# Laying a first MLP, cut into small pieces, under the attention of heads 9 to 32

## The chip, the cores and the metric

One core of a Trainium2 chip runs the whole program. The metric is device time in microseconds (us) of one execution. TensorE (PE) multiplies matrices and transposes, ScalarE (ACT) applies functions and copies, VectorE (DVE) does elementwise work and reductions, GpSimd (POOL) does slower elementwise work in SBUF, and SyncE (SP) issues the DMAs.

## The reference

Three stages follow one another. Heads are 32 (4 batches of 8), each 576 tokens by 64; the MLPs see 2304 tokens of 512.

```python
# attention, per head
scores = scale * (q @ k.T);  bias = -(cum[:, None] - cum[None, :])
scores = where(causal, -1e9, scores + minimum(bias, 0.0))
attn = exp(scores - max(scores));  attn = attn / (sum(attn) + 1e-9)
x = attn @ v                       # heads of a batch side by side: 512 wide
# first MLP (512 -> 1024 -> 512)
h = x @ w_in
solu = h * softmax(h)
ln = (solu - mean) / sqrt(var + 1e-6) * g_ln
x = ln @ w_out
# second MLP (512 -> 2048 -> 512)
h = x @ w_in2
g = h * clip(h + 3, 0, 6) / 6
out = g @ w_out2
```

Everything is float32 and is multiplied as split numbers: each operand is a high part (rounded to PE's fp32r type) and a low part (the rest), and a product is the sum of high*high, high*low and low*high, three matmuls.

## The kernel before, in words

The program has three stages, and each engine has its own instruction stream, written out by hand; semaphores with counts connect them.

**Attention** goes in steps of one head (`step(m, ...)` on every engine, loops over two heads). A head has five query tiles i of 128 rows (the last 64), and tile i has i+1 blocks of keys. In step m PE computes scores of head m+1 (`scores`, L483 high*high and low*high together through stacked q, L487 the causal mask, L489 the low part of k), transposes the probabilities of head m (`transpose_probs`, L502 and L504) and multiplies the transposed probabilities of head m-1 with the values (`weighted_values`, L523: for every key block three passes, v_hi with pT_hi, v_hi with pT_lo, v_lo with pT_hi; v is padded to 128 columns with zeros, so that two heads add up in one PSUM tile). DVE finds the row maximum while it adds the bias (L709), sums of exps get their epsilon (L731) and are inverted (L739), DVE scales the first four tiles of probabilities by them (`normalize`, L724), and makes the low part of the transposed probabilities (L718). ACT makes exps with their sums (L910), scales the last tile (L904), copies the transposed probabilities out of PSUM as the high part (L888), makes the high part of q and k (L894) and copies the finished pair of heads (L917). POOL makes the low parts of q and k (L399, L402), splits v (L408, L410), and w_in in 16 parts (L285, L287). SP loads q and k (L309), the bias row (L312) and v (L315, L316); every raw buffer is there twice, one for even and one for odd heads. Transposed probabilities go through PSUM banks 6 and 7 in turn, and scores through banks 0 to 3.

**First MLP**: 18 tiles of 128 tokens, in `slot(u, ...)`. For each tile ACT and POOL split x (L973, L427), PE makes h (`hidden`, 24 matmuls of 512 columns, L569 to L571) into one of two pairs of PSUM banks, DVE finds its maximum (L791), ACT the exps (L967), DVE the sum's inverse (L801, L804), the product (L806) and the mean (L810), ACT the squares (L961), POOL the inverse root (L433, L436), DVE the normalized rows (L796), PE transposes them (L580, 8 per tile), ACT and DVE split them (L978, L817), and PE projects three tiles at once (`project`, L594 to L596, 384 columns). ACT copies the result (L953).

**Second MLP**: 6 groups of 384 tokens, 16 pieces f each: 12 matmuls of 384 columns (L633 to L635) and 9 of 512 (L649 to L651) per piece.

What sets the order is the code itself: an engine takes its instructions in the order in which the functions issue them, and stands at the first one whose semaphore isn't there yet.

## Time and profile before

| | us |
|---|---|
| runs, median of 3 (lowest, highest) | 916.44 (915.82, 917.17) |
| profiled execution, its own span | 917.3 |
| PE busy | 866.4 (94%), 4864 matmuls |
| DVE busy | 446.7 (49%) |
| ACT busy | 429.9 (47%) |
| POOL busy | 243.6 (27%) |

The span lies within the spread of the runs, so nothing to speak of lies around it. PE's matmuls overlap: a row's duration reaches from an instruction's start to the modelled end of its result, and the next one starts earlier. How fast PE goes is seen from start to start. The busy shares are means over three stages: until 284 us attention, until 512 us the first MLP (with the first pieces of the second among its last tiles), then the second MLP.

### The profile page before, as it was taken

The page shows a single profiled execution, that of the slowest core. Times are in us where ns is not written, and L with a number is a line of the kernel's source. Part 1 is how long each engine was busy: PE and PEld are TensorE (multiplying, and loading weights), DVE is VectorE, ACT ScalarE, POOL GpSimd, SP SyncE. Part 2 cuts the span into 40 slices and gives each one's busy share as a digit, 9 for nine tenths or more (in the row PEclk, how much of TensorE's full clock was granted, in tenths as well). Part 3 has the DMA queues.
Part 4 walks back from the last instruction along what each step waited for, and adds up shares of the span by engine and source line. Part 5 has one row for each costly group of instructions (what it writes and reads, how often), then busy time and mean ns, then how long its engine had stood idle before and what let it go on. Part 6 is the DMA issues. An engine that isn't in the chain of part 4 may idle for free.

```text
span 917.3 us, 15385 instructions
## 1 busy us (share of the span) xinstructions
PE 866.4 (94%) x4864; PEld 766.0 (84%) x4864; DVE 446.7 (49%) x1146; ACT 429.9 (47%) x957; POOL 243.6 (27%) x259
## 2 busy tenths in 40 slices
PE   4988888998898999999999999999999999999997
PEld 3867777777777798998998999999898989999996
DVE  4888898888992835245244222232322332322222
ACT  4878888888883724334233343232322322322222
POOL 4456566665643314234210153000000000000000
PEclk9999999999999999999999999999999999999999
DMA  6955445454424000000000420000000000000000
GB/s 161 275 135 135 123 116 127 130 135 121 115 62 138 1 1 1 1 0 0 0 0 2 148 81 1 35 1 1 35 1 1 34 0 0 34 0 1 35 1 34
DMA packets 25744, 50.92 MB, mean 56 GB/s; under 512 B 5424, under 2 KB 9520, under 8 KB 25712
## 3 DMA queue, kind: packets, MB, share of 16 engines
q1 hardware_dynamic: 25712, 50.50, 19.8%
q8 instruction: 20, 0.33, 0.1%
q14 instruction: 12, 0.10, 0.0%
HBM read 45.69 MB, written 4.79 MB: 55 GB/s over the span
## 4 chain that ended last, share of the span: by engine, by line
PE 71%; ACT 10%; DVE 8%; issue 6%; DMA 2%; SPq 1%; ACTq 0%; DVEq 0%; POOL 0%; POOLq 0%
PE psum L650 7%; PE psum L651 7%; PE psum L635 7%; PE psum L633 7%; PE psum L634 7%; PE psum L649 7%; ACT prob L910 4%; PE psum L594 4%; PE psum L595 4%; PE psum L596 4%; PE psum L569 3%; PE psum L571 3%; PE psum L570 3%; ACT pT_hi L888 2%; DVE prob L709 2%
## 5 line engine op out<-in xcount | busy, mean ns | idle before, releaser
L845 DVE SCALAR_TENSOR_TENSOR act<-act,psum 128x384 f32<-128x384 f32 x96 | 53.1, 554 | 295.8 <-ACT act L1010 295.8
L1010 ACT ACTIVATE act<-psum,three 128x384 f32<-128x384 f32 x96 | 55.8, 582 | 269.0 <-PE psum L635 268.3
L910 ACT ACTIVATE prob<-prob,nmax 128x128 f32<-128x128 f32 (+4 forms) x160 | 96.0, 600 | 40.0 <-DVE nmax L709 40.0
L523 PE MATMUL psum<-pT_hi,v_sp 128*128 128x320 f32 (+3 forms) x448 | 101.3, 301 | 0.0
L709 DVE CUSTOM_DVE_ANT_0 prob<-psum,bias 128x128 f32<-128x128 f32 (+4 forms) x160 | 84.7, 531 | 9.3 <-DMA bias<-cum_dram 7.3
L483 PE MATMUL psum<-qk_st 128*128 128x128 f32 (+2 forms) x192 | 71.2, 379 | 10.6 <-POOL k_lo L402 10.6
L635 PE MATMUL psum<-x_hi,w_late_lo 128*128 128x384 f32 (+1 forms) x240 | 81.0, 337 | 0.0
L633 PE MATMUL psum<-x_hi,w_late_hi 128*128 128x384 f32 (+1 forms) x240 | 80.8, 337 | 0.0
L634 PE MATMUL psum<-x_lo,w_late_hi 128*128 128x384 f32 (+1 forms) x240 | 80.6, 336 | 0.0
L718 DVE TENSOR_TENSOR pT_lo<-psum,pT_hi 128x128 fp32r<-128x128 f32 (+4 forms) x160 | 77.2, 482 | 5.9 <-ACT pT_hi L888 3.2
L489 PE MATMUL psum<-k_lo,qk_st 128*128 128x128 f32 (+2 forms) x192 | 78.9, 411 | 0.0
L523 PEld LDWEIGHTS psum<-pT_hi,v_sp 128*128 128x128 f32 x448 | 76.3, 192 | 2.1
L502 PE MATMUL psum<-ident,prob 128*128 128x128 f32 x320 | 60.3, 288 | 17.5 <-DVE pT_lo L718 16.5
L399 POOL TENSOR_TENSOR qk_st<-qk_raw,qk_st 64x576 fp32r<-64x576 f32 x32 | 45.7, 1430 | 103.0 <-ACT qk_st L894 102.9
L888 ACT ACTIVATE pT_hi<-psum 128x128 fp32r<-128x128 f32 (+4 forms) x160 | 67.8, 424 | 9.4 <-PE psum L502 7.3
L651 PE MATMUL psum<-w_late_hi,g_lo 128*128 128x512 f32 x180 | 71.2, 396 | 0.0
L650 PE MATMUL psum<-w_late_lo,g_hi 128*128 128x512 f32 x180 | 71.1, 395 | 0.0
L649 PE MATMUL psum<-w_late_hi,g_hi 128*128 128x512 f32 x180 | 70.0, 389 | 0.0
L502 PEld LDWEIGHTS psum<-ident,prob 128*128 128x128 f32 x320 | 38.9, 146 | 35.5 <-issue 28.7
L523 PE MATMUL psum<-pT_lo,v_sp 128*128 128x320 f32 (+3 forms) x224 | 68.1, 304 | 0.0
L594 PE MATMUL psum<-lnT_hi,w_out_hi 128*128 128x384 f32 x192 | 64.7, 337 | 1.5 <-DVE lnT_lo L817 1.5
L724 DVE TENSOR_SCALAR prob<-prob,rden 128x128 f32<-128x128 f32 (+3 forms) x128 | 63.4, 496 | 2.3
(98 smaller groups left out, 2088.7 us busy)
## 6 DMA issues: line engine op xcount, KB each, us to landing
qk_raw<-qkT SPq DMA_DIRECT2D x64, 288.0 KB, 4.2
bias<-cum_dram SPq DMA_DIRECT2D x32, 288.0 KB, 4.1
out<-out_sb SPq DMA_DIRECT2D x6, 768.0 KB, 3.5
v_raw<-v_main SPq DMA_DIRECT2D x32, 128.0 KB, 2.0
w_late_raw<-w_in SPq DMA_DIRECT2D x10, 256.0 KB, 3.0
w_late_raw<-w_out SPq DMA_DIRECT2D x10, 256.0 KB, 3.8
w_in_raw<-w_in SPq DMA_DIRECT2D x1, 2048.0 KB, 12.3
w_out_raw<-w_out SPq DMA_DIRECT2D x1, 2048.0 KB, 15.4
```

The source lines that it names most:

```text
L502: last = pe.transpose(bank(ring)[:, j * P:(j + 1) * P], prob[s_ % 2][:, src * P:(src + 1) * P], ident[:, :])
L523: last = pe.matmul(psum[:, O_AT + q0:O_AT + q1], v_sp[p][:, j, v_part, :], pT[p][:, j, q0:q1], start=(p == 0 and k == 0), stop=(p == 1 and ...
L594: pe.matmul(ps, w_out_hi[:, f, cols], lnT_hi[:, f, :], start=(f == 0), stop=False)
L633: pe.matmul(ps, hi[:, cols], xh, start=(c_ == 0), stop=False)
L634: pe.matmul(ps, hi[:, cols], xl, start=False, stop=False)
L635: last = pe.matmul(ps, lo[:, cols], xh, start=False, stop=(c_ == NC - 1))
L649: pe.matmul(bank(4 + k), gh, hi, start=(f == 0), stop=False)
L650: pe.matmul(bank(4 + k), gh, lo, start=False, stop=False)
L651: last = pe.matmul(bank(4 + k), gl, hi, start=False, stop=(f == NF2 - 1))
L709: dve.tensor_tensor_reduce(out=prob[p][:, BLK[i] * P:BLK[i] * P + n], in0=psum[:, at:at + n], in1=bias[p][:, 0:n], scale=-SCALE, scalar=3. ...
L888: sc.activation(pT_hi[s_ % 2][:, 0:i + 1, i * P:i * P + width], ps, ACT.Copy).then_inc(pT_hi_done, 1)
L910: sc.activation(rows, rows, ACT.Exp, scale=-1.0, bias=nmax[:, p, i:i + 1], accum_out=rsum[:, p, i:i + 1]).then_inc(exp_done, 1)
```

## The change

- The attention's parts are now five slots to a head, n = 5m + k, and the first MLP is laid over the same numbering: tile t of it has the ten slots from 45 + 10t on (slot 45 is where the tenth head, m = 9, begins). Slots 0 to 159 hold attention, so tiles 0 to 11 begin beside it, and tiles 12 to 17 come behind it, in the same order of pieces. r = 0 to 9 is the slot within a tile. All loops are written out.
- h has one pair of PSUM banks instead of two, transposed probabilities one bank from slot 45 on, transposed rows and projections share one bank, and scores have three banks. The projection takes two tiles (256 columns) instead of three.
- The probabilities are not divided any more. v_hi and v_lo stand side by side as 128 columns, so a key block takes two passes (pT_hi, pT_lo) instead of three, and the output has the high product in one half of the partitions and the low in the other. ACT copies one half across (`copy_corr`), DVE adds the other (`add_parts`), POOL spreads the inverse sums over 64 columns (`widen`), PE transposes them (`scales`) and DVE multiplies a finished pair by them (`scale_pair`).
- q, k and v have one raw buffer each instead of two.

The diff is cut to the core: layout and numbering, the loads on SP, the spreading on POOL, then PE, DVE and ACT.

```diff
+SLOTS = 5
+TILE_SLOTS = 10
+MOE_FROM = SLOTS * (HEADS + 1)
+MOE_TO = MOE_FROM + TILE_SLOTS * NT
...
+CUTS = ((0, 2 * P), (2 * P, SEQ))
+SCORE_GROUPS = ((0, 1), (2,), (3,), (4,))
+SCORE_AT = (0, P, BANK, 2 * BANK, 2 * BANK - 288 - 512)
+PJW = 2 * P
+NPJ = NC * (NT // 2)
+H_CUTS = (0, 5, 10, 15, 20, 24)
...
-        qk_raw = [sb(a, f"qk_raw{p}", [P, 2, SEQ]) for p in range(2)]
-        v_raw = [sb(a, f"v_raw{p}", [P, NQ, DH]) for p in range(2)]
+        qk_raw = sb(a_region, "qk_raw", [P, 2, SEQ])
+        v_raw = sb(a_region, "v_raw", [P, NQ, DH])
...
+        O_BANK = 4
+        H_BANK = 5
+        L_BANK = 7
+        h_ps = psum[:, H_BANK * BANK:H_BANK * BANK + F1]
+        def turn(m, i):
+            n = SLOTS * m + i
+            return 3 if n % 2 == 0 or n >= MOE_FROM else L_BANK
...
+            def load_qk(h):
+                wait(sp, q_lo_done, h)
+                wait(sp, k_lo_done, h)
...
+            for m in range(-1, NH):
+                if 2 <= m + 2 < NH:
+                    load_bias(m + 2)
+                if m + 3 < NH:
+                    load_qk(m + 3)
+                if m + 2 < NH:
+                    load_v(m + 2)
...
+            def widen(h):
+                pool.wait_ge(rden_done, h + 1)
+                wait(pool, scale_ready, 2 * (h // 2))
+                pool.tensor_copy(wide[:, :, h % 2, :], rden[:, h % 2, :].unsqueeze(2).broadcast_to([P, NQ, DH])).then_inc(wide_done, 1)
...
+            def transpose_probs(m, i):
+                pe.wait_ge(exp_done, NQ * m + i + 1)
+                n = SLOTS * m + i
+                wait(pe, pT_lo_done, n if n >= MOE_FROM else n - 1)
...
+                q0, q1 = CUTS[c]
+                keys = [j for j in range(NQ) if j * P < q1]
+                for j in keys:
+                    at = max(q0, j * P)
+                    for part, (pA, pB) in enumerate(((pA_hi, pB_hi), (pA_lo, pB_lo))):
+                        pT = pB[:, j, at - q0:q1 - q0] if c else (pA[:, 0:2 * P], pA[:, 2 * P:3 * P])[j]
+                        last = pe.matmul(psum[:, O_BANK * BANK + at - q0:O_BANK * BANK + q1 - q0],
+                                         v_sp[h % 2][:, j, :, :].rearrange("p a d -> p (a d)"), pT,
+                                         start=(j == 0 and part == 0), stop=(j == keys[-1] and part == 1))
+                last.then_inc(pv_done, 1)
...
+            for n in range(-SLOTS, MOE_TO):
+                m, k = n // SLOTS, n % SLOTS
+                t, r = (n - MOE_FROM) // TILE_SLOTS, (n - MOE_FROM) % TILE_SLOTS
+                if 0 <= m < NH:
+                    transpose_probs(m, k)
+                if k < 4 and m + 1 < NH:
+                    scores(m + 1, k)
+                if k == 1 and 1 <= m <= NH:
+                    weighted_values(m - 1, 1)
+                if k == 3 and 0 <= m < NH:
+                    weighted_values(m, 0)
+                if t >= 0:
+                    if r in (1, 2) and t >= 1:
+                        transpose_ln(t - 1, r - 1)
+                    if r < 5:
+                        hidden(t, r)
+                    if 3 <= r < 9 and t >= 2:
+                        project(2 * (t - 2) + (r - 3) // 3, (r - 3) % 3, 3)
+                if k in (0, 2) and m % 2 == 0 and 2 <= m <= NH:
+                    scales(m // 2 - 1, k // 2)
...
+            def add_parts(h, c):
+                row, col, tok = tokens(h)
+                q0, q1 = CUTS[c]
+                dve.wait_ge(corr_done, 2 * h + c + 1)
+                x = xT[row:row + DH, col, tok + q0:tok + q1]
+                dve.tensor_tensor(x, psum[row:row + DH, O_BANK * BANK:O_BANK * BANK + q1 - q0], x, ALU.add).then_inc(sum_done, 1)
...
+            for n in range(-SLOTS, MOE_TO):
+                m, k = n // SLOTS, n % SLOTS
+                t, r = (n - MOE_FROM) // TILE_SLOTS, (n - MOE_FROM) % TILE_SLOTS
+                if m + 1 < NH and k >= 1:
+                    for i in SCORE_GROUPS[k - 1]:
+                        row_max(m + 1, i)
+                if 0 <= m < NH:
+                    split_probs(m, k)
+                    if k == 0:
+                        invert(m)
+                if k == 1 and 1 <= m <= NH:
+                    add_parts(m - 1, 1)
+                if k == 3 and 0 <= m < NH:
+                    add_parts(m, 0)
+                if t >= 0:
+                    if r in (1, 2) and t >= 1:
+                        split_ln(t - 1, r - 1)
+                    if r == 5:
+                        max1(t)
+                    if r == 6:
+                        solu(t)
+                    if r == 8:
+                        norm(t)
+                    if t == 0 and r < NF1:
+                        split_w_out(r)
+                    if t == NT - 1 and r in (3, 4, 7, 9):
+                        split_x2(0, (3, 4, 7, 9).index(r))
+                if k in (0, 2) and m % 2 == 0 and 2 <= m <= NH:
+                    scale_pair(m // 2 - 1, k // 2)
...
+            for n in range(-2 * SLOTS, MOE_TO):
+                m, k = n // SLOTS, n % SLOTS
+                t, r = (n - MOE_FROM) // TILE_SLOTS, (n - MOE_FROM) % TILE_SLOTS
+                if 0 <= m < NH:
+                    copy_probs(m, k)
+                if k == 0 and m + 2 < NH:
+                    split_qk(m + 2)
+                if 0 <= m + 1 < NH and k >= 1:
+                    for i in SCORE_GROUPS[k - 1]:
+                        exp_row(m + 1, i)
+                if k == 1 and 1 <= m <= NH:
+                    copy_corr(m - 1, 1)
+                if k == 3 and 0 <= m < NH:
+                    copy_corr(m, 0)
+                if t >= 0:
+                    if r in (1, 2) and t >= 1:
+                        copy_ln(t - 1, r - 1)
+                    if r == 5:
+                        exp1(t)
+                    if r == 7:
+                        square(t)
+                    if t >= 2 and r in (6, 9):
+                        copy_x2(2 * (t - 2) + r // 9)
+                    if t == 0 and r < NF1:
+                        split_w_out(r)
+                    if t == NT - 1 and r in (3, 4, 7, 9):
+                        split_x2(0, (3, 4, 7, 9).index(r))
+                if t >= -1 and r == 9 and t + 1 < NT:
+                    split_x(t + 1)
```

Three places of the instruction order, with their semaphore waits.

**DVE, attention with the heads one after another, before.** L709 is the row maximum, L724 the scaling of probabilities, L718 the low part of the transposed ones.

```order
L709 ISA prob,nmax<-psum,bias 128x256 [waits scores_ready]
L709 ISA nmax 128x1
L735 REGISTER_ALU
L61 REGISTER_ALU [waits den_done]
L739 RECIPROCAL rden<-den 128x2 [waits norm_last_done,norm_done]
L724 TENSOR_SCALAR prob<-prob,rden 128x512 [waits rden_done]
L714 REGISTER_ALU
L718 TENSOR_TENSOR pT_lo<-psum,pT_hi 128x2x128 [waits pT_hi_done]
```

and **after, from slot r = 6 of a tile on.** L667 is `add_parts`, L691 to L699 are `solu`, L640 is the row maximum, L651 the low part, L675 `scale_pair`.

```order
L667 TENSOR_TENSOR xT<-psum,xT 64x320 [waits corr_done]
L691 TENSOR_SCALAR den<-esum 128x1 [waits exp1_done]
L693 RECIPROCAL rden<-den 128x1 [waits den1_done]
L695 SCALAR_TENSOR_TENSOR es,solu_sum<-psum,rden,es 128x1024 [waits rden1_done]
L699 TENSOR_SCALAR neg_mu<-solu_sum 128x1 [waits solu_done]
L640 ISA prob,nmax<-psum,bias 128x384 [waits scores_ready]
L640 ISA nmax 128x1
L651 TENSOR_TENSOR pB_lo<-psum,pB_hi 128x3x128 [waits pT_hi_done]
L675 TENSOR_TENSOR xT<-psum,xT 128x320 [waits sum_done,scale_ready]
L640 ISA prob,nmax<-psum,bias 128x512 [waits scores_ready]
```

The scalings (L724) are gone; between the row maxima and low parts of the attention now stand the addition, which waits for ACT's copy, and the first MLP's `solu`, which waits for ACT's exps.

**PE, transposes and scores, before.** L502 and L504 are transposes of probabilities, L523 the product with the values.

```order
L483 MATMUL psum<-qk_st 128x128 [waits max_done]
L487 MATMUL psum<-mask_bf,ident_bf 128x128
L489 MATMUL psum<-k_lo,qk_st 128x128
L61 REGISTER_ALU [waits norm_last_done]
L504 MATMUL psum<-ident,prob 128x64 [waits pT_lo_done]
L504 MATMUL psum<-ident,prob 128x64 x4
L523 MATMUL psum<-pT_hi,v_sp 128x64
L523 MATMUL psum<-pT_lo,v_sp 128x64
L523 MATMUL psum<-pT_hi,v_sp 128x64
```

and **after, over the end of slot r = 9 of a tile and r = 0 of the next.** L465 are transposes of probabilities, L451 to L455 scores, L512 is `hidden`.

```order
L465 MATMUL psum<-ident,prob 128x64 [waits pT_lo_done,exp_done]
L465 MATMUL psum<-ident,prob 128x64 x4
L465 MATMUL psum<-ident,prob 128x128 [waits pT_lo_done,exp_done]
L451 MATMUL psum<-qk_st 128x128 [waits max_done,k_lo_done,q_lo_done]
L453 MATMUL psum<-mask_bf,ident_bf 128x128
L455 MATMUL psum<-k_lo,qk_st 128x128
L451 MATMUL psum<-qk_st 128x256
L453 MATMUL psum<-mask_bf,ident_bf 128x128
L455 MATMUL psum<-k_lo,qk_st 128x256
L512 MATMUL psum<-w_in_hi,xs_hi 128x512 [waits sq_done,xs_lo_done]
```

Nothing stands between two transpose groups there, and each waits (pT_lo_done) for the low part of the group just before it; behind the scores comes the next tile's first `hidden`, which waits for POOL's part of x (xs_lo_done).

**SP, the loads of a head, before:**

```order
L309 ISA [waits qk_lo_done]
L309 DMA qk_raw<-qkT 64x1152 x2
L61 REGISTER_ALU
L312 ISA [waits max_done]
L312 DMA bias<-cum_dram 128x576
```

and **after:**

```order
L286 DMA bias<-cum_dram 128x576 [waits max_done]
L282 DMA qk_raw<-qkT 64x1152 [waits k_lo_done,q_lo_done]
L282 DMA qk_raw<-qkT 64x1152
L290 DMA v_raw<-v_main 128x256 [waits v_lo_done]
L291 DMA v_raw<-v_tail 64x64
```

They look alike, but with one buffer the load of head h now waits for POOL's split of head h-1, where it waited for that of head h-2.

## Rows read from the trace of the kernel before

**Rows 1.** Windows in attention and second MLP: us, busy (instructions) per engine, clock, DMA share, GB/s

```profile
core 0: us, PE busy (x) PEld busy (x) DVE busy (x) ACT busy (x) POOL busy (x), PEclk, DMA share, GB/s
150.00:200.00 50.00, 44.91 (x328) 37.39 (x327) 44.61 (x140) 42.04 (x108) 30.66 (x32) 1.00 0.48 124
...
700.00:800.00 100.00, 100.00 (x504) 90.57 (x503) 29.28 (x56) 28.51 (x58) 0.00 (x0) 1.00 0.04 16
```

**Rows 2.** Timeline of one head: start us, us, engine, line, operation [idle before]

```profile
151.24 0.57 ACT L888 ACTIVATE pT_hi<-psum 128x512 fp32r<-128x512 f32 x1
...
152.74 1.16 ACT L894 ACTIVATE qk_st<-qk_raw 128x1152 fp32r<-128x1152 f32 x1
152.80 0.74 DVE L709 CUSTOM_DVE_ANT_0 prob<-psum,bias 128x576 f32<-128x576 f32 x1
...
153.47 0.48 DVE L718 TENSOR_TENSOR pT_lo<-psum,pT_hi 128x320 fp32r<-128x320 f32 x1
...
153.89 0.28 PE L523 MATMUL psum<-pT_lo,v_sp 128*128 128x192 f32 x1
...
153.97 1.53 POOL L399 TENSOR_TENSOR qk_st<-qk_raw,qk_st 64x576 fp32r<-64x576 f32 x1 [2.34 <-ACT qk_st L894]
154.00 0.33 PE L523 MATMUL psum<-pT_hi,v_sp 128*128 128x192 f32 x2
...
154.78 0.74 DVE L731 TENSOR_SCALAR den<-rsum 128x2 f32<-128x2 f32 x1 [0.35 <-ACT prob L910]
...
155.57 1.54 POOL L402 TENSOR_TENSOR k_lo<-qk_raw,qk_st 128x576 fp32r<-128x576 f32 x1
```

**Rows 3.** Groups by form, exps: busy us, mean ns | idle before

```profile
L910 ACT ACTIVATE prob<-prob,nmax 128x512 f32<-128x512 f32 x32 | 22.7, 710 | 0.0
...
L910 ACT ACTIVATE prob<-prob,nmax 128x128 f32<-128x128 f32 x32 | 12.7, 397 | 4.2 <-DVE nmax L709 4.2
```

**Rows 4.** Timeline, second MLP: PE from start to start

```profile
700.38 0.39 PE L649 MATMUL psum<-w_late_hi,g_hi 128*128 128x512 f32 x1
...
700.61 0.40 PE L650 MATMUL psum<-w_late_lo,g_hi 128*128 128x512 f32 x1
```

**Rows 5.** Tile qk_raw, 120 to 200 us: issue to landing

```profile
DMA to landing us min/median/max: 3.5/4.2/4.6
```

**Rows 6.** Timeline: first bias load; SP's answer to POOL

```profile
10.07 0.82 SPq L312 DMA_DIRECT2D bias<-cum_dram  x2
...
157.79 0.87 POOL L410 TENSOR_TENSOR v_sp<-v_raw,v_sp 128x320 fp32r<-128x320 f32 x1
...
158.91 0.34 SPq L315 DMA_DIRECT2D v_raw<-v_main  x1
```

**Rows 7.** Page, DMA issues: KB, us to landing

```profile
w_in_raw<-w_in SPq DMA_DIRECT2D x1, 2048.0 KB, 12.3
```

**Rows 8.** Timeline, the first MLP's chain in two tiles

```profile
341.02 0.14 DVE L801 TENSOR_SCALAR den<-esum 128x1 f32<-128x1 f32 x1
...
341.50 1.28 DVE L806 SCALAR_TENSOR_TENSOR solu<-psum,rden,e_sb 128x1024 f32<-128x1024 f32 x1
...
346.33 0.62 ACT L973 ACTIVATE xs_hi<-xT 128x512 fp32r x1
...
347.22 1.30 POOL L427 TENSOR_TENSOR xs_lo<-xT,xs_hi 128x512 fp32r<-128x512 f32 x1 [6.96 <-ACT xs_hi L973]
...
351.34 1.23 DVE L791 TENSOR_REDUCE nmax<-psum 128x1 f32<-128x1024 f32 x1 [2.58 <-PE psum L571]
...
352.60 1.12 ACT L967 ACTIVATE e_sb<-psum,nmax 128x1024 f32<-128x1024 f32 x1 [3.54 <-DVE nmax L791]
```

**Rows 9.** Timeline: PE around two gaps

```profile
311.41 0.39 PE L571 MATMUL psum<-w_in_hi,xs_lo 128*128 128x512 f32 x1
...
313.68 1.60 PE L580 MATMUL psum<-ident,solu 128*128 128x128 f32 x8 [1.89 <-DVE lnT_lo L817]
...
496.36 0.44 PE L594 MATMUL psum<-lnT_hi,w_out_hi 128*128 128x384 f32 x1 [1.48 <-DVE lnT_lo L817]
```

**Rows 10.** Window behind the first of these gaps

```profile
312.00:318.00 6.00, 4.32 (x16) 3.61 (x17) 5.34 (x10) 4.47 (x9) 2.55 (x4) 0.72 0.01 1
```

More of the change, by code:

```diff
@@ L37 @@
 KW = [min((i + 1) * P, SEQ) for i in range(NQ)]
+ROWS = [min(P, SEQ - i * P) for i in range(NQ)]
 INV_SCALE = float(DH) ** 0.5
@@ new lines, in build, with weight_chunk @@
+        xs_lo = sb(first, "xs_lo", [P, NC, P], F32R)
+        first.close()
+        a_region.close()
+        second = ExitStack()
+        w2_hi = [None] * NF2
+        w2_raw = [None] * NF2
+        w2_lo = [None] * NF2
+        def weight_chunk(f):
+            w2_hi[f] = sb(second, f"w2_hi{f}", [P, WT], F32R)
+            with nc.sbuf_tensor(f"w2_raw{f}", [P, WT], F32) as raw:
+                w2_raw[f] = raw
+            w2_lo[f] = sb(second, f"w2_lo{f}", [P, WT], F32R)
+        for f in range(EARLY):
+            weight_chunk(f)
@@ new lines, in scales @@
+            def scales(pair, c):
+                pe.wait_ge(wide_done, 2 * pair + 2)
+                pe.wait_ge(sum_done, 4 * pair + 3 + c)
+                q0 = CUTS[c][0]
+                tiles = ((0, 1), (2, 3, 4))[c]
+                for i in tiles:
+                    w = ROWS[i]
+                    at = O_BANK * BANK + i * P - q0
+                    last = pe.transpose(psum[:, at:at + w], wide[0:w, i, :, :].rearrange("p a d -> p (a d)"), ident[0:w, 0:w])
+                last.then_inc(scale_ready, 1)
@@ new lines, in hidden @@
+            def hidden(t, part):
+                if part == 0:
+                    if t == 0:
+                        pe.wait_ge(w_in_split, W_IN_PARTS)
+                    pe.wait_ge(xs_lo_done, t + 1)
+                    wait(pe, sq_done, t)
+                for n in range(H_CUTS[part], H_CUTS[part + 1]):
+                    half, c_, term = n // 12, n % 12 // 3, n % 3
+                    x = (xs_hi, xs_hi, xs_lo)[term][:, c_, :]
+                    w = (w_in_hi, w_in_lo, w_in_hi)[term][:, c_, half * BANK:(half + 1) * BANK]
+                    last = pe.matmul(bank(H_BANK + half), x, w, start=(n % 12 == 0), stop=(n % 12 == 11))
+                if part == len(H_CUTS) - 2:
+                    last.then_inc(h_ready, 1)
@@ new lines, in transpose_ln @@
+            def transpose_ln(t, part):
+                if part == 0:
+                    pe.wait_ge(ln_done, t + 1)
+                    pe.wait_ge(pT_lo_done, MOE_FROM)
+                    wait(pe, x2_done, min(2 * max(t - 1, 0), NPJ))
+                wait(pe, lnT_lo_done, 2 * t + part)
+                for j in range(4):
+                    f = 4 * part + j
+                    last = pe.transpose(bank(L_BANK)[:, j * P:(j + 1) * P], es[t % 2][:, f * P:(f + 1) * P], ident[:, :])
+                last.then_inc(lnT_ready, 1)
@@ new lines, in project @@
+            def project(q, part, parts):
+                g, d = q // NC, q % NC
+                if part == 0:
+                    if q == 0:
+                        pe.wait_ge(w_out_lo_done, NF1)
+                    pe.wait_ge(lnT_lo_done, 4 * (g + 1))
+                    if q % 2 == 0 and q < NPJ - 4:
+                        pe.wait_ge(lnT_lo_done, 2 * (q // 2 + 2))
+                    wait(pe, x2_done, q)
+                cols = slice(d * P, (d + 1) * P)
+                for n in range(24 * part // parts, 24 * (part + 1) // parts):
+                    f, term = n // 3, n % 3
+                    w = (w_out_hi, w_out_hi, w_out_lo)[term][:, f, cols]
+                    x = (lnT_hi, lnT_lo, lnT_hi)[term][g % 2][:, f, :]
+                    last = pe.matmul(bank(L_BANK, PJW), w, x, start=(n == 0), stop=(n == 23))
+                if part == parts - 1:
+                    last.then_inc(x2_ready, 1)
@@ L859, in copy_out @@
                 dve.tensor_copy(out_sb[:, 1, :], bank(5)).then_inc(out_copied_dve, 1)
-            def group(g):
+            for g in range(NG):
                 for f in range(NF2):
```

971 lines of the change are left out of this document (368 added, 603 removed).

## The prediction

> **What bounds the kernel now.** I read the windows first, then timelines. In attention [rows 1] PE, DVE and ACT are all busy 84 to 90% of the time and none is full, so the order in which they hand work on sets the pace; in the second MLP PE alone is full. The 504 matmuls of that window are 24 pieces of 21, so a piece takes 100/24 = 4.17 us. A head has 53 matmuls (12 for scores, 5 masks, 15 transposes, 21 products), so the 328 of the first window are 6.2 heads, 8.1 us each. The timeline of one head [rows 2] shows how to cost the two middle engines. DVE's row maximum lasts 0.74 but the next instruction starts 0.67 behind it: each DVE or ACT instruction takes about 0.1 less than its duration from its own engine, while another engine waits for all of it plus 0.03 to 0.12. An exp takes its full mean, 0.40 to 0.71 for 128 to 512 columns [rows 3], since a read of its sum follows.
>
> **What PE gains.** Two passes instead of three remove 7 of 21 matmuls a head. A matmul of 192 columns or less takes 0.11 us from start to start [rows 2]; in proportion up to the 0.23 of 512 columns [rows 4], 256 takes 0.12 and 320 takes 0.145. The products fall from 2.65 to 1.77 us a head, 28 us over 32 heads. A head needs 6.0 us of PE then (transposes 1.57, scores with masks 2.39, products 1.77, scales 0.27). A tile of the first MLP needs 24 x 0.23 (hidden), 8 x 0.105 (transposes) and 48 x 0.12 (projection in 256 columns, before 32 of 384 at 0.175), 12.0 us. Two heads and a tile would take 24.0 us if PE were never idle; before, they take 2 x 8.1 + 12.0 = 28.2 (24 x 0.23, 32 x 0.175 and 8 x 0.105 make 12.0, PE full). So there are 4.2 us to win for each tile that is overlaid, 48 for eleven and a half, if nothing new waits.
>
> **First heads, alone: slower.** With one raw buffer, loading and splitting q and k is a ring: ACT's copy 1.16, hand-over 0.07, POOL 1.43 and 1.54 with 0.17 between [rows 2], landing 4.2 after its issue, 3.5 to 4.6 [rows 5], SP's answer 0.25 behind POOL and 0.56 for the first of two issues [rows 6]: 9.4 us a head. The chain of DVE and ACT alone gives 8.1, so the ring decides. The first bias issue is at 10.07 [rows 6]; q and k of head 1 follow at 10.5 to 11.1, land at 15.3, and one ring later, 24.7, the first regular head begins. Nine heads take 84.6. The two weights of 2 MB, 12.3 us each to landing [rows 7], fall into this stretch on the same queue; between nothing and 12 each I take 5 together, since POOL's splitting of w_in waits too. Slot 45 comes at 24.7 + 84.6 + 5 = 114.3. At 8.1 a head it would come 12 sooner.
>
> **Tile and two heads overlaid.** I follow one tile's ten slots from the start of the first transposes. *First part, 2.66 us:* ACT is still at the exp of slot 9 (0.28 more), copies a projection (0.28) and splits x (0.62), POOL takes 0.07 + 1.29 and PE 0.12 more [rows 8]; `hidden` waits for that, and all behind it. *Second, PE's own work to slot 5, 13.15:* hidden 5.5, transposes of probabilities 1.46, scores 1.7, products 1.76, transposed rows 0.84, projection 1.9. *Third, slots 5 to 9, 13.76:* here ACT and DVE wait for each other. Transposes and copy 0.6, low part 0.21, inverses 0.42, maximum of h 1.26, exp of h 1.10, copy 0.29, two exps 0.89, the copied half 0.45, addition 0.40, `solu` 1.9 (0.14, 0.16, 1.28 and hand-overs), row maximum 0.59, exp 0.62, squares 1.14, copy 0.47, exp 0.71, half 0.39, addition 0.33, norm 0.72, row maximum 0.67, low part 0.60 [rows 2, 3, 8]; an operation without a row of its own is scaled by its columns from the rows of its engine, an estimate. The sum passes ACT's copy of the half into DVE's addition, behind which the next row maximum stands, and from there back to ACT's exp: four times in five slots. PE has 9.3 us of work there and waits for the rest, with gaps of about 1.4, 2.0 and (in the first part) 1.85 us. A tile is 29.6.
>
> **Two surcharges.** The small scaling of sums on DVE lasted 0.74, ending as POOL's instruction ended [rows 2], where the first MLP's equal lasts 0.14 with POOL idle [rows 8]. In slot 6 the same kind of instruction meets POOL's splits: 0.6 more, 30.2. The Trainium skill (SBUF — State Buffer, Who interferes with whom) says that GpSimd and VectorE share a port pair as an exclusive lock; with that rule the row agrees. PE's clock was full in 150 to 200 us [rows 1], with short gaps. After a gap of 1.9 us (start to start 2.27) eight transposes took 1.60, which is the 1.2 GHz level; after 1.48 the next matmul took 0.44, the 2.4 GHz level [rows 9]. The 6 us around the first had a mean of 0.72, which costs 6 x 0.28 = 1.7 us [rows 10]. Gaps here lie at that border, so I take half, 0.75 a tile, between 0 and 1.7. The Trainium skill (TensorE: Matmul & The Clock Gate, A second HAM failure mode) warns of a PE that idles briefly between groups and pays at each return to full clock; by it every tile would pay, 15 x 1.7 = 26 instead of 11.
>
> **The first two tiles** have no projection, but DVE and ACT split w_out (8 parts of 0.6): 51 for both. Tiles 2 to 10 take 9 x 30.95 = 278.6. Tile 11's first half runs beside the last head, 15.8, the rest 8.5.
>
> **Tiles 12 to 17, alone.** One pair of banks for h makes a ring. Hidden, transposed rows, the first projection piece, a wait of 0.4 for the shared bank and the matmul's own latency make 8.0 (5.5 + 0.84 + 0.95 + 0.4 + 0.3); then come maximum 1.26, exp 1.10, copy of a projection 0.38 (it stands behind the exp) and 0.1, three projection pieces 2.85 and 0.2, copy 0.28, split of x 0.62 and 1.48 on POOL: 16.3, where PE has 12.0 and before, with two pairs of banks, takes no more than that. PE's gap before the next hidden is 2.6. Six of them 97.8, clock 4.5, less 2.6 at the last.
>
> **Second MLP.** 96 x 4.17 = 400.3, then four projections (96 x 0.12), the last tile's transposes and their wait, 13.7 (before, this stood in the first MLP), and 5.5 for the last outputs, as now. Three edits I cost at nothing. The widening on POOL is hidden by POOL's idle time, 39% of the window [rows 1]; without it, it would lengthen the ring by its own 0.6 us. The transposed scales are counted in PE's 6.0. The splits of the late weights each stand beside a piece of 4.17 us, as before; if they came late, PE would wait for the seventh piece.
>
> **Sum.** 114.3 + 51 + 278.6 + 15.8 + 8.5 + 99.7 + 400.3 + 13.7 + 5.5 = 987 us, against the span of 917.3; the median of the runs lies 0.9 below it, so 986.
>
> **Rivals.** (1) *Faster:* ACT and DVE run ahead far enough in the single streams that PE stays full. The mechanism is the filling of slots 5 to 9 (PE idle 4.5 there) and of the wait for x. For it: DVE is busy 0.89 of 8.1 us a head [rows 1], 14.5 for two, and the tile adds some 5.5 [rows 8], so of 30 us it has 10 free. Against it: each wait named above is in instruction order. Both stretches at PE's 24.0 and 12.5 give 986 - 9 x 6.95 - 6 x 4.5 = 897. It decides from 25.5 us for an overlaid tile and 13.5 for a lone one; from there the kernel is faster than before. The Trainium skill (Perfetto Trace Analysis, Optimization Strategy) says that regimes with different contended engines may gain by interleaving; that is this rival. (2) *Half of the waits gone* (27 and 14.5 a tile, ring of 8.8): 986 - 36 - 11 - 5 = 934. (3) *Clock low in most of each tile's first part:* PE's 13.15 and 8.0 grow by a third or more, 986 + 9 x 3.5 + 6 x 3 = 1035. For it: the gap row; against it: attention at full clock with gaps. (4) That it doesn't do what it says: the order shows the pieces interleaved and two passes, so no chance.
>
> **How the numbers follow.** Forecast 55%, half of the waits 15%, clock 18%, faster 12%. The forecast's own bounds: 3.5 to 4.6 for landing (7 us), weights 0 to 24, clock 0 to 1.7 a tile, 1 us either way in an overlaid tile (10) and in a lone one: 955 to 1020. The range of 8 in 10 reaches to half of the waits and to the middle of the clock case: 922 to 1030. A measurement of this kernel can tell 0.2%, 1.8 us, from no change; hardly any case lies within it: faster 0.11, same 0.02, slower 0.87.
>
> **What would show it.** Right: attention rings of 9.4 us and slot 45 near 114 us; ACT waiting for DMA before its copy of q and k; an overlaid tile near 30 us with PE waiting for DVE's low parts and for POOL's part of x; a lone tile near 16 with PE waiting for `sq_done` and POOL; mean clock below 1.00 there. Wrong: PE full from slot 45 on, or the first heads at 8 us.

## The result, and the profile after

| | before | after |
|---|---|---|
| median of the runs, us | 916.52 | 1034.18 |
| profiled execution, span | 917.3 | 1036.5 |
| PE / DVE / ACT / POOL busy | 866 / 447 / 430 / 244 | 904 / 425 / 436 / 247 |

The changed kernel is slower: ratio 1.1265, 95% interval 1.121 to 1.132, about 116 us. The forecast was 986 with 922 to 1030; the direction was right, the time 48 us too low and just outside the range. The four runs spread from 1027.1 to 1038.6 us, and the profiled one is the slowest of them, so its stretches are at the long end.

Windows of the changed kernel: first heads alone, as [rows 1], tiles overlaid, lone tiles, second MLP.

```profile
core 0: us, PE busy (x) PEld busy (x) DVE busy (x) ACT busy (x) POOL busy (x), PEclk, DMA share, GB/s
27.00:117.00 90.00, 70.22 (x405) 59.03 (x403) 51.57 (x164) 59.04 (x151) 56.45 (x77) 0.79 0.54 146
150.00:200.00 50.00, 39.77 (x201) 32.31 (x202) 28.13 (x73) 28.35 (x69) 18.41 (x22) 0.73 0.24 63
200.00:450.00 250.00, 216.75 (x1365) 188.43 (x1362) 141.23 (x376) 141.29 (x343) 82.50 (x98) 0.89 0.24 63
...
508.00:600.00 92.00, 70.40 (x419) 60.01 (x418) 27.12 (x47) 25.12 (x49) 35.27 (x42) 0.96 0.07 25
700.00:800.00 100.00, 100.00 (x504) 90.67 (x503) 28.29 (x56) 28.25 (x58) 0.00 (x0) 1.00 0.05 16
```

No engine is full before the second MLP. In 150 to 200 us PE went through 6.6 matmuls a us before, at a granted clock of 1.00, and goes through 4.0 now, at 0.73; many of those of now are longer, so the busy share, 90% before and 80% now, is the fairer comparison. The second MLP is what it was, 504 matmuls in 100 us.

ACT's copy of q and k begins each head, so its starts are a ruler: head 2, slot 45, the ends of tiles 0 and 1, and the start of tile 10; then the exps of h of the first two lone tiles.

```profile
24.62 1.16 ACT L787 ACTIVATE qk_st<-qk_raw 128x1152 fp32r<-128x1152 f32 x1 [4.90 <-DMA qk_raw<-qkT]
...
119.66 1.15 ACT L787 ACTIVATE qk_st<-qk_raw 128x1152 fp32r<-128x1152 f32 x1
...
158.28 1.15 ACT L787 ACTIVATE qk_st<-qk_raw 128x1152 fp32r<-128x1152 f32 x1
...
189.04 1.15 ACT L787 ACTIVATE qk_st<-qk_raw 128x1152 fp32r<-128x1152 f32 x1
...
452.70 1.15 ACT L787 ACTIVATE qk_st<-qk_raw 128x1152 fp32r<-128x1152 f32 x1
...
523.34 1.11 ACT L831 ACTIVATE es<-psum,nmax 128x1024 f32<-128x1024 f32 x1 [4.86 <-DVE nmax L686]
...
540.04 1.11 ACT L831 ACTIVATE es<-psum,nmax 128x1024 f32<-128x1024 f32 x1 [4.83 <-DVE nmax L686]
```

Set against the prediction's sum (the second MLP's first matmul starts at 615.0):

| stretch | predicted | measured | difference |
|---|---|---|---|
| to head 2 | 24.7 | 24.6 | -0.1 |
| nine heads alone, with weights | 89.6 | 95.0 | +5.4 |
| tiles 0 and 1 | 51 | 69.4 (38.6 + 30.8) | +18.4 |
| tiles 2 to 9, eight | 8 x 30.95 | 8 x 32.96 | +16.1 |
| tile 10 to the second MLP | 155.0 | 162.3 | +7.3 |
| second MLP | 419.5 | 421.5 | +2.0 |

Together +49.1 on 987. How an overlaid tile goes is seen in tile 6. First PE at its start, the timeline:

```profile
319.31 0.30 PE L465 MATMUL psum<-ident,prob 128*128 128x128 f32 x1 [1.68 <-DVE pB_lo L651]
...
321.85 0.80 PE L512 MATMUL psum<-w_in_hi,xs_hi 128*128 128x512 f32 x1 [1.52 <-POOL xs_lo L399]
322.44 0.63 PE L512 MATMUL psum<-w_in_lo,xs_hi 128*128 128x512 f32 x1
322.87 0.63 PE L512 MATMUL psum<-w_in_hi,xs_lo 128*128 128x512 f32 x1
...
328.73 0.39 PE L512 MATMUL psum<-w_in_lo,xs_hi 128*128 128x512 f32 x1
328.96 0.39 PE L512 MATMUL psum<-w_in_hi,xs_lo 128*128 128x512 f32 x1
...
338.12 0.27 PE L465 MATMUL psum<-ident,prob 128*128 128x128 f32 x1
```

Then the chain of waits from the first transposes of slot 5 (start us, us, what):

```profile
338.27 0.12 PE psum L465
...
339.24 1.20 DVE nmax L686
...
340.46 0.55 ACT es L831
...
342.83 0.44 ACT xT L814
...
343.29 0.50 DVE xT L667
...
344.20 1.30 DVE es L695 x2
```

Both gaps of PE were forecast: one behind DVE's low part, one behind POOL's part of x. After them a matmul of 512 columns goes from start to start in 0.43 us (322.44 to 322.87) until about 327.8, then in 0.23 (328.73 to 328.96), as in [rows 4]: 5.9 us at the 1.2 GHz level, which at half speed is 3.0 us lost. From `hidden` to slot 5 PE takes 16.3 us (321.85 to 338.12), where 13.15 were forecast. The chain from slot 5 on passes maximum, exp, ACT's copied half, DVE's addition and `solu` in the forecast order.

### The profile page after: what moved, and what is told of

Same layout as the page of the kernel before. It is cut to its first block, busy times and chain, and to the rows that moved or that the text cites. A ratio compares the mean times of both kernels' runs of the same rounds, so it can differ in the third digit from the quotient of the medians.

```text
span 1036.5 us, 13705 instructions
## 1 busy us (share of the span) xinstructions
PE 904.2 (87%) x5008; PEld 793.6 (77%) x5008; DVE 425.2 (41%) x1038; ACT 436.2 (42%) x985; POOL 247.4 (24%) x291
## 4 chain that ended last, share of the span: by engine, by line
PE 67%; ACT 8%; issue 8%; DVE 7%; POOL 5%; DMA 4%; SPq 0%; ACTq 0%; POOLq 0%; DVEq 0%
PE psum L512 11%; PE psum L561 7%; PE psum L563 7%; PE psum L578 6%; PE psum L562 6%; PE psum L579 6%; PE psum L577 6%; PE psum L543 6%; PE psum L485 4%; DMA qk_raw<-qkT 2%; PE psum L465 2%; POOL xs_lo L399 2%; DVE nmax L686 2%; ACT prob L795 2%; PE psum L525 2%
## 5 line engine op out<-in xcount | busy, mean ns | idle before, releaser
L561 PE MATMUL psum<-x_hi,w_hi 128*128 128x384 f32 x384 | 129.5, 337 | 1.9 <-DVE x_lo L716 1.9
L563 PE MATMUL psum<-x_hi,w_lo 128*128 128x384 f32 x384 | 129.6, 337 | 0.0
L562 PE MATMUL psum<-x_lo,w_hi 128*128 128x384 f32 x384 | 129.0, 336 | 0.0
L465 PE MATMUL psum<-ident,prob 128*128 128x128 f32 (+1 forms) x480 | 84.4, 289 | 35.6 <-DVE pB_lo L651 28.5
L579 PE MATMUL psum<-w_hi,g_lo 128*128 128x512 f32 x288 | 113.9, 396 | 0.0
L578 PE MATMUL psum<-w_lo,g_hi 128*128 128x512 f32 x288 | 113.7, 395 | 0.0
L577 PE MATMUL psum<-w_hi,g_hi 128*128 128x512 f32 x288 | 112.0, 389 | 0.0
L543 PE MATMUL psum<-lnT_hi,w_out_hi 128*128 128x256 f32 x288 | 84.5, 293 | 20.0 <-ACT xT L849 20.0
L451 PE MATMUL psum<-qk_st 128*128 128x128 f32 (+2 forms) x192 | 80.3, 423 | 23.4 <-DVE nmax L640 10.6
L465 PEld LDWEIGHTS psum<-ident,prob 128*128 128x128 f32 (+1 forms) x480 | 57.2, 154 | 52.8 <-issue 34.6
L512 PE MATMUL psum<-w_in_hi,xs_hi 128*128 128x512 f32 x144 | 66.3, 461 | 31.2 <-POOL xs_lo L399 31.2
L640 DVE CUSTOM_DVE_ANT_0 prob<-psum,bias 128x128 f32<-128x128 f32 (+4 forms) x160 | 83.3, 536 | 10.6 <-PE psum L455 9.9
L543 PE MATMUL psum<-lnT_lo,w_out_hi 128*128 128x256 f32 x288 | 83.9, 291 | 0.0
L455 PE MATMUL psum<-k_lo,qk_st 128*128 128x128 f32 (+2 forms) x192 | 83.3, 434 | 0.0
L543 PE MATMUL psum<-lnT_hi,w_out_lo 128*128 128x256 f32 x288 | 83.1, 289 | 0.0
## 6 DMA issues: line engine op xcount, KB each, us to landing
w_in_raw<-w_in SPq DMA_DIRECT2D x1, 2048.0 KB, 11.9
```

Source lines behind the costliest of these rows:

```text
L455: last = pe.matmul(ps, q, k_lo[p][:, lo_:hi_], start=False, stop=True)
L465: last = pe.transpose(ps[:, j * w:(j + 1) * w], prob[m % 2][0:w, src:src + P], ident[0:w, 0:w])
L512: last = pe.matmul(bank(H_BANK + half), x, w, start=(n % 12 == 0), stop=(n % 12 == 11))
L543: last = pe.matmul(bank(L_BANK, PJW), w, x, start=(n == 0), stop=(n == 23))
L561: pe.matmul(ps, w2_hi[f][:, cols], xh, start=(c_ == 0), stop=False)
L562: pe.matmul(ps, w2_hi[f][:, cols], xl, start=False, stop=False)
```

## The experiments

Ratios are to the kernel before on the same chip. The difference to the changed kernel is (ratio - 1.1265) x 916.5; it is uncertain by some 7 us, as both intervals are about 5 us wide to each side; the pace of a single stretch is read from the traces. An idle matmul is one whose result nobody uses.

| run | ratio, 95% | us against changed |
|---|---|---|
| e1 serial | 1.1711 [1.1663, 1.1759] | +41 |
| e2 x in slot 8 | 1.0856 [1.0798, 1.0914] | -37 |
| e3 second q/k buffer | 1.1152 [1.1098, 1.1207] | -10 |
| e4 additions later | 1.1062 [1.1013, 1.111] | -19 |
| e5 idle matmuls in tiles | 1.0969 [1.0919, 1.1018] | -27 |
| e6 w_out spread | 1.1185 [1.1127, 1.1243] | -7 |
| e7 no second half | 1.0923 [1.0881, 1.0964] | -31 |
| e8 idle matmuls in heads | 1.1273 [1.1229, 1.1318] | +1 |
| e9 = e3 + e7 | 1.083 [1.0805, 1.0855] | -40 |
| e10 = e3 + e4 + e6, x in slot 6 | 1.0359 [1.0341, 1.0376] | -83 |
| e11 = e2 + e3 + e4 + e6 | 1.0527 [1.0501, 1.0552] | -68 |
| e12 = e10 + e8 | 1.0439 [1.0412, 1.0467] | -76 |
| e13 serial, two buffers | 1.1545 [1.1498, 1.1591] | +26 |
| e14 serial, no second half | 1.1493 [1.145, 1.1536] | +21 |
| e15 serial, both | 1.1074 [1.1032, 1.1115] | -18 |
| e16 = e13 + idle matmuls | 1.1762 [1.1714, 1.181] | +46 |
| e17 = e10 + e7 | 1.0295 [1.0237, 1.0353] | -89 |

### e1: nothing beneath the attention

```diff
-MOE_FROM = SLOTS * (HEADS + 1)
+MOE_FROM = SLOTS * (NH + 1)
...
-                    pe.wait_ge(pT_lo_done, MOE_FROM)
+                    pe.wait_ge(pT_lo_done, NQ * NH)
```

> The first tile starts after the last head instead of at slot 45; nothing runs beneath the attention. Theory A (the overlay itself loses time, by its waits): attention goes near the old pace of 8.2 us a head, 25 + 30 x 8.2 = 271 us, then 18 tiles of 16.7 (300), then 421 and 13: about 1005, faster than the changed kernel. Theory B (the overlay does win time, and the new attention and the lone tile with one pair of banks are slow by themselves): heads stay at 9.9 us up to the last, 320 to 330 us, then 300, then 421: 1045 to 1065, slower than the changed kernel.

Theory B's order came, with a slightly longer total than it gave (1075 us for 1045 to 1065). Heads 11 to 31 take 9.65 us each, and 18 lone tiles 17.2 each, where the kernel before has 8.2 and 11.9 (nine tiles from the exp of h at 358.93 to that at 466.01: 107.1 / 9). So the overlay itself wins about 41 us; what loses is that each of its two parts is slower in the new form.

### e2: x of the next tile one slot earlier

```diff
-                if t >= -1 and r == 9 and t + 1 < NT:
+                if t >= -1 and r == 8 and t + 1 < NT:
                     split_x(t + 1)
```

The same on ACT and POOL.

> The split of x for the next tile one slot earlier (r = 8 instead of 9) on ACT and POOL. Chain theory: PE's wait for POOL's part of x (1.5 to 2.8 us a tile) goes, in the overlaid tiles and in part in the lone ones: 11 x 1.5 + 6 x 1.3 = 24 us less, 1010; if the low clock behind that gap goes with it, up to 3 more a tile, 980. Capacity theory (ACT, DVE and PE are simply full together, order doesn't matter): 1034, unchanged.

PE's waits, 189 to 380 us, of the changed kernel:

```profile
PE psum L543 <- ACT xT L849: 8.6, 6, 1.4
PE psum L465 <- DVE pB_lo L651: 8.4, 5, 1.7
PE psum L512 <- POOL xs_lo L399: 7.7, 6, 1.5
```

and of e2:

```profile
PE psum L465 <- DVE pB_lo L651: 10.1, 6, 1.7
PE psum L543 <- ACT xT L849: 10.0, 7, 1.4
```

The wait for x is gone, the clock between 190 and 450 us is 0.96 instead of 0.89, and tiles 2 to 9 last 29.3 each instead of 33.0. The wait was 1.3 to 1.5 a tile; the rest of the 3.7 goes with the clock. Within e2 tiles 2 to 9 come in two lengths, 28.3 and 29.8 to 29.9, and only in the longer ones did the level fall. Lone tiles stay at 16.0 to 17.1: POOL's split stands there behind its variance.

### e3 and e4: a second raw buffer; additions one slot later

e3 gives heads 1 to 9 two raw buffers in turn, the second where the transposed rows come later, and loads head 1 at once. e4:

```diff
-                if k == 1 and 1 <= m <= NH:
+                if k == 2 and 1 <= m <= NH:
                     add_parts(m - 1, 1)
-                if k == 3 and 0 <= m < NH:
+                if k == 4 and 0 <= m < NH:
                     add_parts(m, 0)
```

> A second raw buffer for q and k of heads 1 to 9 (it lies where a buffer of the first MLP begins to be used at slot 76). Ring theory: the heads before slot 45 come at 8.1 to 8.5 us instead of 9.9, slot 45 at about 105 instead of 120 us, 1019 in all. Rival (the chain of ACT and DVE, or the weight loads, hold these heads at the same pace): no change at 1034.

> DVE's addition of the copied half one slot later (k = 2 and 4 instead of 1 and 3). Chain theory: DVE no longer stands waiting for ACT's copy before it makes the next row maximum, about 0.8 us at each of four places of a tile, of which two are on the chain: 1.6 to 3 us a tile and up to 1 a head before, 1000 to 1015. Capacity theory: unchanged, 1034.

In e3 head 2 begins at 17.3, 7.3 earlier, and slot 45 at 107.5, 12.2 earlier; nine heads take 90.2, 10.0 each. That is 5 us less than in the changed kernel's profile, but e2 and e6, which leave these heads as they are, take 90.9 and 91.6 there: the earlier start is the gain, and the pace hardly moved. The ring is not all that holds them. In e4 tiles 0 and 1 take 63.5 instead of 69.4 and tiles 2 to 9 32.3 each instead of 33.0, less than the 1.6 to 3 a tile that were expected. DVE no longer stands at the copied half (32.1 us in eight tiles, 2 to 9, of the changed kernel), but waits more for ACT's copies of probabilities and rows.

### e5: ten idle matmuls in each of tiles 1 to 11

```diff
+                if covered and r == 0:
+                    fill(t, 5)
                 if 0 <= m < NH:
                     transpose_probs(m, k)
                 if k < 4 and m + 1 < NH:
                     scores(m + 1, k)
+                if covered and r == 0:
+                    fill(t, 5)
```

`fill` issues matmuls of 512 columns into the free bank of h, in PE's two gaps.

> Ten more matmuls of 512 columns a tile (tiles 1 to 11) in PE's two gaps at the tile's start, five before the transposes of slot 0 and five behind its scores; their result is overwritten. Clock theory: PE stays at its upper level, the first part of a tile takes 13.3 instead of 16.4 us, up to 3 us a tile less, 1004 us, though 26 us of work are added. Rival (the low clock isn't what lengthens the tile, or gaps aren't what lowers it): 1034 to 1045.

The window of 189 to 380 us:

```profile
189.00:380.00 191.00, 178.46 (x1193) 152.62 (x1193) 116.62 (x308) 117.40 (x287) 69.71 (x82) 1.00 0.28 70
```

More work, less time: the clock is 1.00 and a tile 30.3, 2.7 less than without. All of it lies in the part between `hidden` and slot 5: 13.6 us in e5's tile 3 (217.37 to 230.93) instead of 16.3, while slots 5 to 9 stay at 13.95. So the clock is most of the 3.1 us by which tile 6 exceeded the forecast there, and the step that priced it at 0.75 a tile failed.

### e6: w_out in every second slot of tiles 0 and 1

```diff
-                    if t == 0 and r < NF1:
-                        split_w_out(r)
+                    if t in (0, 1) and r % 2 == 0 and r < 8:
+                        split_w_out(4 * t + r // 2)
```

> The eight parts of w_out are split in every second slot of tiles 0 and 1 up to slot 6, four in each, and not in eight slots of tile 0. Tile 0 takes 38.6 us and tile 1 30.8 in the changed kernel. Theory A (the chain of ACT and DVE is full in tile 0 and each part costs it about 1 us wherever it stands): tile 0 gets 4 us shorter and tile 1 4 longer, total same within 2 us. Theory B (each part pushes a wait only where slots 5 to 7 are crowded by the maximum, exp and solu of h): the two together get 3 to 5 us shorter, about 1031.

Tile 0 takes 32.4, tile 1 33.2: the two 3.8 less than 69.4, on theory B's side. The total is 7 less, which its uncertainty of 7 doesn't tell from 3.8.

### e7, e8, e9: what holds the first heads

e7 leaves out the contribution of v's low part: ACT doesn't copy, DVE copies the first half instead of adding. e8 puts nine idle matmuls into each of heads 1 to 8. e9 is e3 with e7.

```diff
-                dve.wait_ge(corr_done, 2 * h + c + 1)
+                dve.wait_ge(pv_done, 2 * h + c + 1)
```

> The contribution of the low part of v is left out: ACT no longer copies the second half of the product's bank, and DVE copies the first half instead of adding it. This takes two ACT instructions a head out of the chain ACT, DVE, next row maximum, ACT's exp. Theory A (this hand-over, four times in five slots, is what holds overlaid tiles and heads): the first nine heads go from 10 to about 9 us, an overlaid tile from 33 to about 30.5, in sum about 40 us less, 995. Theory B (the time is PE's low clock and the waits for x and the shared transposition bank): under 15 us less, 1020 or more.

> Nine idle matmuls of 512 columns are added to each of heads 1 to 8, three behind each of the first three score groups, into banks that nothing else uses yet. PE's mean granted clock there was 0.84 and lower, a head took 10 us. Theory A (the heads' pace is set by PE at a low clock because of its gaps): clock to 0.95 or more, heads at 9 us or less, slot 45 at 110 instead of 119.7, whole about 1027. Theory B (the chain through DVE and ACT sets the pace and the clock only follows): the fillers add their own 2 us a head or part of it, slot 45 at 122 to 135, whole 1037 to 1050.

> Two edits together: the second raw buffer of q and k for heads 1 to 9, and the contribution of the low part of v left out (no copy of the second half by ACT, no addition by DVE). Each by itself left the first nine heads at 10 us. Theory A (two bounds of nearly the same length stand there, the loading ring of 9.4 us and the hand-overs between PE, ACT and DVE of about 9.7): only both edits together shorten a head, to 8.5 to 9 us, slot 45 at 93 to 98, and the whole is 25 us below the run with the second part left out alone, about 980. Theory B (something else, PE's low clock or the weight loads, holds the heads at 10): slot 45 near 107 again, about 992.

Nine heads take 90.9 in e7, as in e2, and 93.8 in e8 (clock 0.91 there instead of 0.79): neither makes them shorter. e7's 31 us come from the overlaid tiles, 30.2 instead of 33.0, as theory A had it there. In e9 slot 45 comes at 103.9, 3.6 before e3's: between the two theories, while the total, 992.9, is theory B's. One of its heads lasts 15.2 us: q and k landed 12.0 us after their issue, behind w_out's load. Weight loads blurred the answer, so the question went to clean heads.

### e13 to e16: heads by themselves, no weights

All are e1 with the edits described above, the second buffer for all heads and the idle matmuls for all from head 1 on.

> The version with nothing beneath the attention (1075 us; heads 10 to 31 at 9.65 us each), with a second raw buffer of q and k for all heads. Theory A (the loading ring of about 9.4 us alone holds a head): heads at 8.2 to 8.7, about 1075 - 12 - 22 = 1041. Theory B (the hand-overs PE, ACT, DVE, row maximum, scores are as long): 9.3 to 9.65, 1060 to 1070. Theory C (both at once): as B here, and only e15 goes below 9.

> The same serial version with one raw buffer, without the contribution of v's low part (no copy of the second half, no addition). Theory A (ring): heads at 9.4 to 9.65, 1067 to 1075. Theory B (hand-overs): 8.9 or less, below 1060. Theory C: as A here.

> Serial, second raw buffer for all heads, and without the contribution of v's low part. Theory A (ring alone): same as with the second buffer alone, within 3 us. Theory B (hand-overs alone): same as with the low part left out alone, within 3 us. Theory C (two bounds of nearly one length): below 9 us a head, 15 us or more below either alone, 1035 to 1045.

> Serial, second raw buffer for all heads, and nine idle matmuls of 512 columns in each head from 1 on. Theory A (the granted clock, 0.84 to 0.88 there, stretches the products from 1.3 to 2.3 us inside the chain): clock 0.95 or more, heads about 0.7 us shorter than without the fillers, 15 to 20 us less in all. Theory B (the fillers cost what the clock gives): within 5 us of it or slower.

| | us a head, 11 to 31 | clock, 150 to 280 us |
|---|---|---|
| e1 | 9.65 | 0.87 |
| e13 second buffer | 9.42 | 0.87 |
| e14 no second half | 9.42 | 0.95 |
| e15 both | 8.00 | 0.92 |
| e16 second buffer, idle matmuls | 10.23 | 0.96 |

Theory C: two bounds of one length, and only both edits together go below. (The totals of e14 and e15, 1057.6 and 1018.6, lie below the 1067 and 1035 that theory C allowed at least.) The chain of waits of e14 is the predicted ring, nothing else:

```profile
199.83 1.17 ACT qk_st L787
...
201.16 1.41 POOL qk_st L362
...
202.65 1.44 POOL k_lo L364
...
204.15 0.47 SPq L282
...
204.66 5.12 DMA qk_raw<-qkT
...
209.80 1.17 ACT qk_st L787
```

That of e13 goes round PE, ACT and DVE instead, twice a head through the second half (L828 and L680 are the copy and the addition in this kernel, L653 the row maximum, L498 the product with the values, L809 the exp):

```profile
201.46 2.31 PE psum L498 x10
203.79 0.45 ACT xT L828
...
204.26 0.48 DVE xT L680
204.74 0.47 DVE prob L653
...
205.25 0.71 ACT prob L809 x2
...
207.17 0.38 ACT xT L828
...
207.57 0.43 DVE xT L680
...
208.03 0.75 DVE prob L653
```

e16 raised the clock and lost 0.8 us a head: the nine idle matmuls stand in that chain. The product of 2.31 here ran at the 1.2 GHz level, and in e10's tiles it takes 1.25, so a fuller clock should shorten the chain (not shown by itself), but this way of getting it costs more than it gives.

### e10, e11, e12, e17: putting it together

e10 and e11 have e3, e4 and e6; e11 splits x in slot 8, e10 in slot 6 where the tokens are ready:

```diff
-                if t >= -1 and r == 9 and t + 1 < NT:
+                if t >= -1 and r == (8 if t + 1 in (0, 4) else 6) and t + 1 < NT:
```

> A version with four edits: second raw buffer of q and k for heads 1 to 9, additions of the parts one slot later, w_out split over tiles 0 and 1, and x of the next tile split in slot 6 (slot 8 for tiles 0 and 4, whose tokens are not ready earlier). Singly the first three gave 12, 19 and 11 us, and splitting x in slot 8 gave 41. Theory A (the gains add, since each is another wait): 1037 - 83 = 954, and the lone tiles lose the 1.3 us of POOL's split between the variance and the next hidden piece, 15.0 instead of 16.7, another 8: 946. Theory B (they overlap, because the chain through slots 5 to 9 is one and the split of x now stands in it): 970 or more.

> The same four edits, but x of the next tile split in slot 8 throughout. Theory A (gains add): 954. Theory B (overlap): 965 to 975. Against the version with slot 6 it tells what the split costs inside the crowded slot 6 and what it saves in lone tiles: if the lone tiles alone differ, this is 8 to 10 us slower.

> The four edits with x in slot 6, and nine idle matmuls of 512 columns in each of heads 1 to 8. With the raw buffer of one head in the way, the fillers raised the granted clock from 0.84 to 0.89 and changed no time. Theory A (with the ring out of the way the clock is in the chain: the values' product lasts 2.3 us instead of 1.3 in it): heads 0.5 to 1 us shorter, 5 to 8 us less than the same version without fillers. Theory B (the fillers take as much of PE as the clock gives back): within 3 us of it.

> The version with four edits (949.5 us; overlaid tile 28.2, heads 9.4 to 10, lone tile 14.6) without the contribution of v's low part, so without ACT's copy and DVE's addition. In the serial versions, with the second raw buffer in, this took 1.4 us off a head. Theory A (the hand-over of the second half is what keeps this version above the kernel before): first heads 1 us shorter each (9), an overlaid tile 26 or less (20): 920 or below. Theory B (with additions a slot later it is hidden, and tiles stand at PE's 24.0 plus the chain of h in slots 5 to 9): 9 to 15 us less, 935 to 940.

The gains nearly add: 10 + 19 + 7 + 37 = 73 singly, 68 in e11; the gap of 5 is within the uncertainty. e10 is 949.51 us, the best complete version here and still 3.6% above the kernel before. In e11 and e10 an overlaid tile is the same, 28.2 for all but the first of tiles 2 to 9, at a clock of 1.00 from 186 us to the lone tiles. Of the 15 us between their medians the traces place 11 in the lone tiles, 16.0 to 17.1 against 14.7. Lines of e10's chain of waits, from `hidden` (L525) past a projection (L556) to the transposes of slot 5 (L478):

```profile
276.65 1.16 PE psum L525 x5
...
289.17 0.94 PE psum L556 x8
290.11 0.12 PE psum L478
```

`hidden` to slot 5 now takes 13.5 us at full clock, against 13.15 forecast; with 0.9 before it and the chain of slots 5 to 9, still 13.9, that makes the 28.2, where PE's own work is 24.0. e12 costs 7 us instead of winning 5 to 8, 4.7 of it before slot 45, where its idle matmuls are. e17 is only 4 to 6 us below e10, less than either theory gave: a tile takes 27.6 instead of 28.2, so with the additions a slot later and the clock full, the second half is nearly hidden in the tiles. Even without it the kernel before is not reached.

## Why the prediction was wrong, and where it was right

The waits that it named are those that stand in tile 6's chain. Two terms of the sum were mis-sized: the clock surcharge of 0.75 us a tile, which measured 3.0 in tile 6, and the 51 us for tiles 0 and 1, which measured 69.4. The stretches that they belong to hold 34.5 of the 49 us. By terms:

- **Start, 24.7:** right to 0.1.
- **First heads, ring of 9.4:** right in size by luck of two equal bounds. "The chain of DVE and ACT alone gives 8.1" took the old chain; the new one carries the copied half and gives 9.4 by itself (e13), and without that half 8.0 (e15). The ring alone gives 9.42 (e14), as forecast. Where both stand the pace is 9.65, and 10.1 to 10.6 with weights.
- **Tiles 0 and 1, 51:** wrong by 18.4, the largest single miss, and given without a sum. The crowding of w_out's parts is 3.8 of it (e6) and DVE's stand at the copied half 5.9 (e4). The mean clock was 0.68 in tile 0 (the window below) and 0.78 in tile 1, which the 51 doesn't name; how much of the rest is the clock's no run shows. With x split earlier and e3, e4 and e6 in, e10 takes 54.8 for both.

```profile
119.66:158.28 38.62, 26.66 (x120) 21.26 (x119) 23.47 (x55) 21.95 (x51) 12.26 (x13) 0.68 0.19 55
```

- **Overlaid tile, 30.95:** its first part, 2.66, measured 2.54 in tile 6 and its third, 13.76, measured 13.96; its PE part, 13.15, measured 16.3. The clock surcharge of 0.75 should have been 3.0: 5.9 us at half speed, where [rows 10] gave 1.7 for the 6 us behind a single gap, and I took about half of that. e5 confirms it: with the gaps filled the same part takes 13.6.
- **Rival 3 (18%, 3.5 a tile, 1035 us):** near in the overlaid tiles, wrong in the lone ones. That its 1035 is the measured 1034 is luck: its 18 us for lone tiles didn't come, and the 18.4 of tiles 0 and 1 are not in it. The Trainium skill (TensorE: Matmul & The Clock Gate, A second HAM failure mode), named there, says that a PE which idles briefly between groups pays at each return to full clock. The trace agrees for the overlaid tiles: the level fell at the start of each of tiles 2 to 10, and in tile 6 it cost 3.0 us, more than the 1.7 that the prediction put on each by that rule. In the lone tiles it agrees only now and then.
- **Port surcharge, 0.6:** the mechanism came, the place was wrong. The small sums behind `solu` never met POOL (0.15 us in all 18 tiles); those of the probabilities did, at a tile's start, where PE waited for POOL's part of x anyway.
- **Lone tile, 16.3 and 0.75 for the clock:** right. Five tiles have a mean of 17.0, four of them 16.7 and one 18.1; only in the one of 18.1 did the level fall.
- **Tile 10 to the second MLP:** +7.3, of the same kind as tiles 2 to 9, with the remainder around the last head; not followed further.
- **Second MLP:** 421.5 for 419.5.
- **Rival 1, faster:** PE all but full in slots 0 to 4 was reached (e10), in slots 5 to 9 never; the tile ends at 28.2, not below 25.5.
- **Slips in the working, of no weight:** a tile's PE work adds up to 12.1 us and not 12.0; POOL's first split of q and k is 1.53 with 0.07 behind it in [rows 2], not 1.43 with 0.17; the copies of q and k in the kernel before are 8.2 us apart, not 8.1.

What stays open: how much of the low clock in the heads alone is cause and how much consequence, since idle matmuls raise it and stand in the chain themselves; and how the rest of the 18.4 us of tiles 0 and 1 divides.

## What to carry to other kernels

Before laying one stage under another, measure each in its new form alone. Here the overlay won 41 us, and the new form that it needed (single buffers, fewer banks, the copied half) cost 157 (e1 against before). Compare the loading ring and the hand-over chain as two separate bounds; when they are equal, removing either shows next to nothing (0.23 us a head each, 1.65 both). And when a producer for the next piece (the split of x) is issued in the last slot, move it earlier first: a gap of 1.5 us cost more in the clock behind it (the rest of e2's 3.7 a tile) than in itself.
